# Attention, mixture of experts and MLP on one core: zeros by another queue, the last block's routing reordered, splits moved

## The reference

```python
for i in range(N):
    e = expert_idx[i]
    if counts[e] < capacity:
        disp[e, counts[e]] = x[i]; pos[i] = counts[e]; counts[e] += 1; keep[i] = True
h = np.maximum(np.einsum('ecd,edf->ecf', disp, w1), 0.0)      # 512 -> 1024
y = np.einsum('ecf,efd->ecd', h, w2)                          # 1024 -> 512
out[i] = gate_w[i] * y[expert_idx[i], pos[i]]                 # kept tokens
```

## Time and profile before

| what | us |
|---|---|
| median of 3 runs | 454.85 |
| the profiled execution, its own time | 452.85 |
| its span | 451.0 |
| PE busy | 434.3 (96%) |
| PE weight loads | 395.1 (88%) |
| DVE busy | 214.2 (47%) |
| ACT busy | 219.7 (49%) |
| POOL busy | 232.0 (51%) |

### The profile page before, as it was taken

One profiled execution on the slowest core, in us unless ns is written; L12 is line 12 of the kernel. 1 busy time (PEld: TensorE's weight loads), 2 busy tenths in 40 slices (PEclk: granted clock), 3 DMA queues, 4 the chain that ended last, 5 costly groups with the idle time before them and its releaser, 6 DMA issues.

```text
span 451.0 us, 8316 instructions
## 1 busy us (share of the span) xinstructions
PE 434.3 (96%) x2928; PEld 395.1 (88%) x2928; DVE 214.2 (47%) x726; ACT 219.7 (49%) x547; POOL 232.0 (51%) x173
## 2 busy tenths in 40 slices
PE   7998899989999999999999999999999999999995
PEld 5786678779999999999999998988999989999983
DVE  4686687786576574764763222231322231312230
ACT  4877688654676576676675543221212222211221
POOL 5004778569988989989899987402000002000002
PEclk9999999999999999999999999999999999999999
DMA  9997992139988768887878200001000001000002
GB/s 175 241 293 196 291 271 69 48 97 331 354 282 285 254 215 264 302 286 253 295 254 278 95 1 0 2 0 70 1 0 0 0 0 70 0 0 0 0 0 76
DMA packets 54247, 63.70 MB, mean 141 GB/s; under 512 B 32064, under 2 KB 32064, under 8 KB 54208
## 3 DMA queue, kind: packets, MB, share of 16 engines
q1 hardware_dynamic: 51392, 58.23, 42.4%
q0 software_dynamic: 1776, 4.73, 2.9%
q10 hardware_dynamic: 1040, 0.26, 0.3%
HBM read 53.76 MB, written 9.44 MB: 140 GB/s over the span
## 4 chain that ended last, share of the span: by engine, by line
PE 76%; POOL 6%; ACT 5%; DVE 4%; DMA 4%; SPq 2%; issue 2%; POOLq 0%; DVEq 0%; ACTq 0%
PE bank L1313 15%; PE bank L1314 14%; PE bank L1315 14%; PE bank L1335 12%; PE bank L1334 6%; POOL w_lo L496 5%; PE bank L1143 3%; ACT prob L625 2%; PE bank L1332 2%; PE bank L1182 2%; SPq L338 2%; PE bank L1160 2%; DMA q_raw<-in_q_dram 2%; PE bank L1194 2%; DMA w_raw<-in_moe_w_dram 1%
## 5 line engine op out<-in xcount | busy, mean ns | idle before, releaser
L496 POOL TENSOR_TENSOR w_lo<-w_raw,w_hi 128x1024 fp32r<-128x1024 f32 x73 | 173.3, 2413 | 17.7 <-DVE w_lo L1063 7.1
L1094 DVE TENSOR_TENSOR bank<-bank,sigmoid 128x384 f32<-128x384 f32 x48 | 27.2, 566 | 135.7 <-ACT sigmoid L747 132.1
L596 POOL DMA_INDIRECT out_dram<-out_stage,permcol x9 | 8.7, 971 | 150.9 <-ACT out_stage L767 147.8
L747 ACT ACTIVATE sigmoid<-bank 128x384 f32<-128x384 f32 x48 | 23.6, 491 | 127.3 <-PE bank L1315 122.4
L655 ACT ACTIVATE w_hi<-w_raw 128x1024 fp32r<-128x1024 f32 x76 | 80.1, 1054 | 3.7 <-DMA w_raw<-in_moe_w_dram 3.7
L1025 DVE TENSOR_REDUCE bank<-bank 128x192 f32<-128x384 f32 (+5 forms) x96 | 49.2, 514 | 42.1 <-PE bank L1335 41.8
L1313 PE MATMUL bank<-x_hi,w_hi 128*128 x192 | 65.0, 338 | 0.7 <-POOL w_lo L496 0.7
L1315 PE MATMUL bank<-x_hi,w_lo 128*128 x192 | 64.6, 336 | 0.0
L1314 PE MATMUL bank<-x_lo,w_hi 128*128 x192 | 64.5, 336 | 0.0
L1335 PE MATMUL bank<-hidden,w_hi 128*128 128x384 f32 (+5 forms) x224 | 62.6, 351 | 0.0
L1313 PE MATMUL bank<-w_hi,g_hi 128*128 128x512 f32 x144 | 56.7, 394 | 0.8 <-DVE g_lo L1098 0.8
(11 more groups left out here) (152 smaller groups left out, 766.4 us busy)
## 6 DMA issues: line engine op xcount, KB each, us to landing
w_raw<-in_moe_w_dram SPq DMA_DIRECT2D x64, 512.0 KB, 6.0
dispatch_dram<-zeros SPq DMA_DIRECT2D x4, 1152.0 KB, 8.6
w_raw<-in_moe_w_in_dram SPq DMA_DIRECT2D x8, 512.0 KB, 4.2
w_raw<-in_moe_w_out_dram SPq DMA_DIRECT2D x8, 512.0 KB, 6.6
dispatched<-dispatch_dram SPq DMA_DIRECT2D x8, 384.0 KB, 7.5
q_raw<-in_q_dram SPq DMA_DIRECT2D x8, 256.0 KB, 6.8
v_raw<-in_v_dram SPq DMA_DIRECT2D x8, 256.0 KB, 5.8
k_raw<-in_k_dram SPq DMA_DIRECT2D x7, 256.0 KB, 8.3
```

Source lines behind the costliest of these rows:

```text
L496: nc.gpsimd.tensor_tensor(wlo[s][:, sl], raw[s][:, sl], whi[s][:, sl], ALU.subtract).then_inc(pool_lo, 1)
L747: nc.scalar.activation(sig[:, f % 2, :], bank[f % 4][:, 0:TB], ACT.Sigmoid).then_inc(sig_ready, 1)
L1094: nc.vector.tensor_tensor(bank[f % 4][:, 0:TB], bank[f % 4][:, 0:TB], sig[:, f % 2, :], ALU.mult).then_inc(gf_ready, 1)
```

## The change

Five parts. (1) The four DMAs of zeros go from SP's queue to POOL's, behind POOL's constants. (2) For the last block DVE makes logits, best expert and one-hot ahead of the slots and gate of block 8; ACT's `gate_exp` goes ahead of `gate_x`; PE waits for the logits' reading behind three of the four `selected` of block 7. The plan is made in another order: `excess` comes first (and releases the branches), offsets and expert order later. (3) During expert 0 ACT splits pieces 1, 2 and 3 of the second expert's weights behind up 5, up 7 and turn 3 (before: up 2, 4, 6). (4) Of the seventh expert (number 6) POOL makes 6 low pieces and DVE 2 (before: 7 and 1). (5) In `last_outputs` (1,13) comes ahead of (0,15).

```diff
@@ -283,7 +283,10 @@
-            return POOLED * e + n + (1 if e > 0 else 0)
+            return sum(map(pooled, range(e))) + n
+
+        def pooled(e):
+            return SPLITS if e == 0 else POOLED - 1 if e == E - 2 else POOLED
@@ -302,6 +305,9 @@
                        ("down", 3): 7}
+        SPLIT_FIRST = {**SPLIT_AFTER, ("up", 5): 1, ("up", 7): 2, ("turn", 3): 3}
+        for late in (("up", 2), ("up", 4), ("up", 6)):
+            del SPLIT_FIRST[late]
@@ -379,11 +385,6 @@
                 load_other_slots(e)
-
-            def empty_slots(e0, n):
-
-                sp.dma_start(disp[e0 * C:(e0 + n) * C, :].rearrange("(n p) d -> p n d", p=SUB),
-                             zeros[0:SUB, :].unsqueeze(1).broadcast_to([SUB, 3 * n, DM])).then_inc(zeroed, 16)
@@ -393,8 +394,6 @@
                 load_qkv(t)
-                empty_slots(2 * (t - 2), 2)
-            empty_slots(2 * NT - 4, E - 2 * NT + 4)
             for t in range(NT, NTOK):
@@ -534,6 +533,13 @@
+            def empty_slots(e0, n):
+                nc.gpsimd.dma_start(disp[e0 * C:(e0 + n) * C, :].rearrange("(n p) d -> p n d", p=SUB),
+                                    zeros[0:SUB, :].unsqueeze(1).broadcast_to([SUB, 3 * n, DM])).then_inc(zeroed, 16)
+
+            pool.wait_ge(zeros_ready, 1)
+            for e in range(0, E, 2):
+                empty_slots(e, 2)
             for t in range(LAST):
@@ -543,7 +549,7 @@
                 if t == 0:
-                    pool.wait_ge(zeroed, 16 * (NT - 1))
+                    pool.wait_ge(zeroed, 16 * E // 2)
                 pool.wait_ge(slot_ready, t + 1)
@@ -571,10 +577,10 @@
-            lows(1, 2, range(POOLED))
+            lows(1, 2, range(pooled(1)))
             for e in range(2, E):
                 pool.wait_ge(dve_lo, e - 1)
-                lows(e, 2 * (e % 2), range(POOLED))
+                lows(e, 2 * (e % 2), range(pooled(e)))
             pool.wait_ge(dve_lo, E - 1)
@@ -697,8 +703,8 @@
             weight_high(1, EARLY + 1 - PIECES, 16)
+            gate_exp(NTOK - 1)
             gate_x(NTOK - 2)
-            gate_exp(NTOK - 1)
             weight_high(1, EARLY + 2 - PIECES, 16)
@@ -715,6 +721,8 @@
                     if t == FC:
+                        if e == 0:
+                            act.wait_ge(plan_ready, 2)
                         off = offset_of(act, e)
@@ -725,7 +733,7 @@
                         nc.scalar.activation(x2hi[:, c, bass.ds(off, w)], bk[:, 0:w], ACT.Copy).then_inc(hi_ready, 1)
-                    p = SPLIT_AFTER.get((kind, c))
+                    p = (SPLIT_AFTER if e > 0 else SPLIT_FIRST).get((kind, c))
                     if p is not None:
@@ -776,7 +784,7 @@
                 x_high(c, FIRST_X[c], FIRST)
-            act.wait_ge(plan_ready, 2)
+            act.wait_ge(plan_ready, 1)
             by_excess(act, rest)
@@ -964,16 +972,16 @@
             place_found(NTOK - 2)
-            slot_found(NTOK - 2)
-            gate_found(NTOK - 2)
             logits_weigh(NTOK - 1, 0)
...
             slot_base(NTOK - 1)
+            slot_found(NTOK - 2)
+            gate_found(NTOK - 2)
             normalize(NTOK - 1, 0)
+            place_found(NTOK - 1)
             gate_found(NTOK - 1)
-            place_found(NTOK - 1)
             slot_found(NTOK - 1)
@@ -988,19 +996,20 @@
                                          ALU.is_gt))
-            start(nc.vector.reduce_sum(rank[:], above[:], axis=AX.X))
-            link(nc.vector.tensor_tensor(kept_above[:], above[:], kept8.unsqueeze(1).broadcast_to(over_e), ALU.mult))
-            start(nc.vector.reduce_sum(off8, kept_above[:], axis=AX.X))
+            link(nc.vector.reduce_sum(rank[:], above[:], axis=AX.X))
             link(nc.vector.tensor_tensor(at_rank[:], rank[:].unsqueeze(1).broadcast_to(over_e),
                                          vals[:, 2, :].unsqueeze(2).broadcast_to(over_e), ALU.is_equal))
-            link(nc.vector.tensor_tensor(ranked[:], at_rank[:].unsqueeze(1).broadcast_to([P, 3, E, E]),
-                                         vals[:].unsqueeze(2).broadcast_to([P, 3, E, E]), ALU.mult))
-            link(nc.vector.reduce_sum(by_rank[:], ranked[:], axis=AX.X))
-            start(nc.vector.tensor_tensor(over8[:], by_rank[:, 0, :], width8[:], ALU.subtract))
-            nc.vector.tensor_copy(plan[:], by_rank[:, 1:3, :]).then_inc(plan_ready, 1)
-            settle()
+            link(nc.vector.tensor_tensor(ranked[:, 0], at_rank[:], kept8.unsqueeze(1).broadcast_to(over_e), ALU.mult))
+            link(nc.vector.reduce_sum(by_rank[:, 0, :], ranked[:, 0], axis=AX.X))
+            link(nc.vector.tensor_tensor(over8[:], by_rank[:, 0, :], width8[:], ALU.subtract))
             link(nc.vector.reduce_max(over[:], over8[:], axis=AX.X))
             nc.vector.tensor_scalar_max(excess[:], over[:], 0.0).then_inc(plan_ready, 1)
+            link(nc.vector.tensor_tensor(kept_above[:], above[:], kept8.unsqueeze(1).broadcast_to(over_e), ALU.mult))
+            link(nc.vector.reduce_sum(off8, kept_above[:], axis=AX.X))
+            link(nc.vector.tensor_tensor(ranked[:, 1:3], at_rank[:].unsqueeze(1).broadcast_to([P, 2, E, E]),
+                                         vals[:, 1:3].unsqueeze(2).broadcast_to([P, 2, E, E]), ALU.mult))
+            link(nc.vector.reduce_sum(by_rank[:, 1:3], ranked[:, 1:3], axis=AX.X))
+            nc.vector.tensor_copy(plan[:], by_rank[:, 1:3, :]).then_inc(plan_ready, 1)
@@ -1050,6 +1059,8 @@
                     if t == FC:
+                        if e == 0:
+                            dve.wait_ge(plan_ready, 2)
                         off = offset_of(dve, e)
@@ -1058,7 +1069,7 @@
                     if e >= 1 and (kind, c) == ("up", 1):
-                        s, sl = 2 * (e % 2) + 1, slice((PIECES - 1) * PIECE, PIECES * PIECE)
+                        s, sl = 2 * (e % 2) + 1, slice((pooled(e) - PIECES) * PIECE, PIECES * PIECE)
                         dve.wait_ge(whi_ready, split_by(e, SPLITS))
@@ -1114,7 +1125,7 @@
-            dve.wait_ge(plan_ready, 2)
+            dve.wait_ge(plan_ready, 1)
             by_excess(dve, rest)
@@ -1283,7 +1294,6 @@
             pe.wait_ge(places_read, NTOK - 1)
-            pe.wait_ge(lg_read, NTOK)
             pe.wait_ge(sel_ready, 1)
@@ -1292,6 +1302,7 @@
             nc.tensor.matmul(bS[1][0][:, 0:E], ones[:], seen[:, NTOK % 3, :], start=True, stop=True).then_inc(count_done, 1)
+            pe.wait_ge(lg_read, NTOK)
             selected(NTOK - 3, KC - 1, True, False)
@@ -1365,10 +1376,8 @@
                         if c == 0:
-                            if e == 0:
-                                pe.wait_ge(pool_lo, SPLITS)
-                            else:
-                                pe.wait_ge(pool_lo, pooled_by(e, POOLED))
+                            pe.wait_ge(pool_lo, pooled_by(e, pooled(e)))
+                            if e > 0:
                                 pe.wait_ge(dve_lo, e)
@@ -1423,8 +1432,8 @@
                 f0, last_f = F2C - FQ, F2C - 1
-                turns = [(0, f) for f in range(f0, last_f)] + [(1, f0), (0, last_f)]
-                turns += [(1, f) for f in range(f0 + 1, F2C)] + [(2, f) for f in range(f0, F2C)]
+                turns = [(0, f) for f in range(f0, last_f)] + [(1, f0), (1, f0 + 1), (0, last_f)]
+                turns += [(1, f) for f in range(f0 + 2, F2C)] + [(2, f) for f in range(f0, F2C)]
                 for t, f in turns:
@@ -1442,7 +1451,7 @@
-            pe.wait_ge(plan_ready, 2)
+            pe.wait_ge(plan_ready, 1)
             by_excess(pe, rest)
```

## The result

| | before | after |
|---|---|---|
| median of the runs, us | 454.77 (451.57 to 455.52, 4 runs) | 462.72 (460.83 to 466.45, 4 runs) |
| profiled execution, us | 452.85 | 462.58 |
| its span, us | 451.0 | 460.5 |
| mean granted clock of TensorE | 0.998 | 0.985 |

After over before is 1.0216 in the comparison of the runs, with a 95% interval of 1.0172 to 1.026 (the two medians alone give 1.0175): slower without doubt, by 1.7 to 2.6%. The prediction was 452.1 us, in a range of 450.8 to 456.5. It missed by 10.6 us and had the sign wrong. What came is its first rival, and of that the case with a chance of 0.05.

A forecast was written before the change was run, and what follows sets the result against it. PE, 76% of the span, was taken to bound the kernel. 452.85 - 1.5 - 0 - 1.25 - 0 - 0 = 450.1 us for the profiled execution; with 2.0 added for the median of the runs, 452.1, range 450.8 to 456.5.

The forecast's parts named there:

- first rival: At block 3's turn of q, zeros crowd out the loads: 458.5 us at a share of 0.25; chance 0.20.
- the case with a chance of 0.05: Within the first rival: loads get next to nothing until all zeros are through, 459.4 us; chance 0.05.
- the share: Loads' part of the DMA engines beside early zeros: at 0.39 nothing waits, at 0.31 the whole gain is gone.
- The rival's own price: Block 3's q at 29.4 us, 7.3 us late, if loads got next to nothing during the zeros: 459.4; chance 0.05.
- The gain of 1.5 for the zeros: At the turns of q of blocks 5 and 6, 1.5 of 1.7 us of PE's DMA waits go.
- The last block, 0: Last block to first expert: expert 0 starts some 0.3 us earlier, lost waiting for the last rows; 0 net.
- The second expert's pieces, 1.25: At expert 0's first down step, later splits of the second expert's pieces take 1.25 us off.
- A piece from POOL to DVE, 0: Behind expert 6's pieces POOL still restarts at 216.88; the MLP start's 0.70 us wait stays; 0 gained.
- (1,13) ahead of (0,15), 0: At each MLP block's end, the 0.68 us stall is before (0,14), ahead of the swapped pair; 0 gained.

The follow-up runs named there:

- zeros_act: The changed kernel with the four zero writes on ScalarE's queue, behind its first exponentials; 462.33 us, one run.
- act_small: The changed kernel with the zeros on ScalarE's queue, each write cut into four by column quarter, in rows of 512 B; 475.89 us.
- zeros_late: The changed kernel with POOL waiting until block 4's v has landed before it issues the zeros; 461.16 us, 1.0169 of before.
- busy: The changed kernel with 42 products that nobody reads on PE ahead of block 2's turn of k; median 462.55 us.
- spread: turns_last with the fourth zero write on SP's queue behind the loads of block 5 instead of ahead; 451.22 us, 0.993 of before.
- splits_only: The kernel before with only the later splits of the second expert's pieces; 454.2 us, 1.0001 of before.
- turns_last: The changed kernel with zeros back on SP, (1,12) and (1,13) ahead of (0,14), and DVE's extra piece from the last expert; 450.9 us, 0.9943 of before.
- no_plan: turns_last without the part on the last block (steps and plan in before's order); 450.62 us, 0.9911 of before.

## Why the prediction was wrong

**The zeros: the step that failed is the share.** The prediction had the right question, the price of zeros on a queue of their own, and the right arithmetic for it: with 0.39 of the engines for the loads nothing waits, with 0.31 the gain is gone. It then took the loads' share from rows 6, where they had 74.5% beside POOL's queue; measured were 11 to 19% from 12 to 28 us, and a wait of 9.0 us where the sum had none. In the window of rows 6 POOL's queue had 96 packets against 1297, from scatters of 128 rows; that is no share for two queues that are both kept full. (How full POOL's was there the trace doesn't show; one for one, it would have been empty for most turns.) The prediction wrote that very objection down ("POOL had only short bursts queued there") and still put 0.05 on the case. The rule of the Trainium skill (DMA: Bandwidth & Descriptors, Queues, rings and completion order), that an engine takes its queues in turn packet by packet, was set aside as not borne out by rows 6. The traces bear it out: 85 to 85 packets from 22 to 23 us in after, 586 to 585 in zeros_act, 1672 to 1665 in act_small, with the exceptions told above (more loads in some windows of after, 311 to 36 in zeros_late). That page of the Trainium skill speaks of packets of several descriptors; what goes one for one here are the packets that the profile counts, 256 B on SP's queue and one row on ScalarE's. The packet sizes were in the rows: 0.33 MB in 96 packets are 3.4 KB, 0.35 MB in 1297 are 0.27 KB.

**The rival's own price** was 7.3 us at block 3's q, for 459.4. The wait came one load sooner, at block 2's k, and q was 11.3 us late, not 7.3. The rival let the loads run at 228 GB/s once the zeros were through; the windows have 221 from 24 to 28, most of it still zeros, and 146 from 28 to 32. And it had no term for the clock, 1.9 us by busy.

**The gain of 1.5 for the zeros** was there in place (11.3 us late at block 3, 9.8 at block 6, but 10.3 again at block 7), and spread shows that it is no gain of the median: 1.7 us of waits from one execution were taken for a constant.

**The last block, 0:** right, and for the reason given: the lead at the start, 0.66 us in other traces where 0.3 was forecast, is spent in a longer wait for the last rows. In after PE is 10.3 us late at block 7's q, 9.98 at expert 0's first product (109.92), and 10.5 at the turns (119.98).

**The second expert's pieces, 1.25:** 1.14 in the trace of after, nothing that the median of splits_only shows. The size in one trace was right; that every execution has it to gain was taken for granted.

**A piece from POOL to DVE, 0:** right. POOL's last restart behind DVE is at 226.19, 9.31 after 216.88, with a longer wait, and PE's wait at the MLP's start is still 0.67 us:

```profile
226.19 50.48 POOL L495 TENSOR_TENSOR w_lo<-w_raw,w_hi 128x1024 fp32r<-128x1024 f32 x21 [3.49 <-DVE w_lo L1074]
...
253.21 0.44 PE L1324 MATMUL bank<-x_hi,w_hi 128*128 x1 [0.67 <-POOL w_lo L495]
```

**(1,13) ahead of (0,15), 0:** right, and turns_last shows the reason to be the true one. The stall stands before (0,14) in after too:

```profile
313.45 0.19 PEld L1324 LDWEIGHTS bank<-w_hi,g_hi 128*128 128x128 f32 x1 [0.68 <-DVE g_lo L1109]
```

## What to carry to other kernels

Before bulk writes go to a second queue, compare the packet sizes of the two, not their bytes: here the queues took turns packet by packet for most of the time, and loads of 256-B packets got a tenth to a fifth of the engines beside packets of 2 to 4 KB, and 40% beside packets of 0.5 KB. In one queue the order protects what is needed first; a second queue takes that order away. A share read where one queue has only short bursts is no share for two full ones. And a small wait, read in one execution, is to be looked for in a second trace before its removal is counted.

## What the runs showed of the hardware

- A full second queue holds up the engine that issues on the first one. SP's issue of block 3's q, 256 KB, took 10.77 us in after, against 0.51 in before, where no issue of a load in the first 50 us took more than 4.76.
- Packets on ScalarE's queue had the length of a row (2.0 KB, 0.5 KB when cut). On GpSimd's they did not follow it: 3.9 KB with rows of 2 KB, 3.1 KB with rows of 512 B.
- Two queues with work went near one for one in packets, whatever their size: 586 to 585 (zeros_act) and 1672 to 1665 (act_small) in 4 us, 85 to 85 in 1 us of after. The loads had more at times (385 to 57) and, just behind queued zeros, almost none (36 to 311 in zeros_late).
- After PE stood still for 9 us its granted clock was at half (1.2 GHz), and 0.77 on average even from 28 to 32 us, where PE was busy again. Products of no use kept it at 1.00 and bought 1.85 us. In turns_last a wait of 2.26 us was followed by a clock of 0.50 from 112 to 116 us. In no_plan it was 0.51, 0.50 and 0.71 in the three windows from 92 to 104 us, with PE busy for 3.74, 4.00 and 4.00 of each 4 us.
